# Loading q and k once each, four projection products of 192 columns, and a rewritten order for the first head: an attention and mixture-of-experts kernel on one core

## The chip, the cores and the metric

The kernel runs on one core of a Trainium2 chip. The metric is the device time of one execution in microseconds (us); lower is better. The engines are named as in the profile: PE (matrix products) with its weight loads PEld, DVE (vector), ACT (scalar, activations), POOL (GpSimd) and SP (the queue that issues most DMA transfers).

## The reference, cut to what matters

```python
# q, k, v: (2, 8, 768, 64); proj: (64, 6)
q_bits = (einsum('bhsd,dk->bhsk', q, proj) > 0)      # 6 sign bits for each row
k_bits = (einsum('bhsd,dk->bhsk', k, proj) > 0)
mask   = q_bucket[:, :, :, None] == k_bucket[:, :, None, :]    # bucket = the 6 bits as a number
scores = where(mask, scale * q @ k.T, -1e9)
attn   = softmax(scores);  x = attn @ v              # 16 heads
x = moe(x)       # each token: its best of 8 experts, relu(x @ w1) @ w2, times two gates
out = elu(x @ w_in) @ w_out
```

## The kernel before, in words

Attention runs head by head (16 heads of 768 rows and 64 dimensions), then comes the routing of the tokens, the expert layers and a last feed-forward block. The change is in the attention alone.

**One head.** q and k arrive transposed, 64 dimensions on the partitions, 768 rows along the free axis. Each is loaded twice, to partitions 0 to 63 and to 64 to 127 of `raw` (`load_qk`, L402; four DMAs a head). `project` (L1143) multiplies the 64 low partitions by `proj_w`: four products of 384 columns, each to its own 32 partitions of PSUM bank `bank_a` (q first half, q second half, k first half, k second half). `sign` (L841, DVE) turns this into 0/1 `bits`. `code` (L1159, PE) multiplies the bits by the +1/-1 `pat_bf`, once for q (c=0) and once for k (c=1), 384 columns each; a bucket matches where the sum equals a popcount. `mask_even` (L847, DVE) and `mask_odd` (L627, ACT) write this match as 64 more rows of the operands `q_a` and `k_a`, so that the score product itself gives about 2^60 less where buckets differ. The products are made of a high part (rounded to fp32r) and a low part (the rest): `high` (L823, DVE) rounds q and k into `q_b` and `k_b`; POOL scales k in `raw` (L532), copies the high parts to the top of `q_a` and `k_a` (L505, L514) and subtracts for the low parts (L507, L516). `scores` (L1168) is four products for one tile of 128 rows, tile m to `pair_s` or `pair_t`.

**The order of the work.** Every engine has its order written out by hand, in groups n; a head has three groups (part = 0, 1, 2), each with two score tiles. In group n PE makes `scores` of tiles m_s and m_s+1, and transposes the exponentials (`turn_exps`, L1184) of tiles m_e = m_s-2 and m_e+1, six 128x128 blocks each: three to the first bank of `pair_u`, which wait until ACT has copied the tile before (`copy_t0`, L647), and three to the second, which wait for DVE's copy (`copy_t1`, L855). Parts 0 and 1 also hold half of the product with v (`times_v`, L1195, 12 products), part 2 holds `last` (L1224) and `project` of the next head. Before the change `code(g, 0)` stands at the end of part 0 and `code(g, 1)` in part 1 between the first `turn_exps` and `times_v`.

DVE's order in a group is

```python
copy_t1(m_e - 1); row_max(m_s); row_max(m_s + 1); copy_t1(m_e)
# part 0: sign(g)      parts 0, 1: high(g + 1, part); mask_even(g, part)
# part 1: inverse(g - 2)
```

and ACT's is

```python
copy_t0(m_e - 1)       # part 0: copy_rows(g - 3)
copy_t0(m_e); exp_rows(m_s); exp_rows(m_s + 1)
# parts 0, 1: mask_odd(g, part)     part 1: copy_u(g - 2)
# heads 8 to 15, parts 0, 1: first_hi(g - 8, part)   (half a chunk of expert weights rounded)
```

**The first head.** Tiles 0 to 5 and their preparation are written out apart. PE bridges its waits with `warm_up` products (`WARM_UP = (7, 10)`, L1246): 7 before `project(0)`, 10 between `code(0, 1)` and `scores(0)`. SP issues q of head 0, proj, the pattern table `pat`, head 1, v, and the remaining constants `cst`; ACT issues k of head 0 (twice) and `first`.

Of the kernel before, what the change touches and what calls it, by code (L numbers as in the profile page):

```python
# [22 lines left out]
ALU = mybir.AluOpType  # L23
ACT = mybir.ActivationFunctionType
AX = mybir.AxisListType
F32 = mybir.dt.float32
# [29 lines left out]
HALF = S // 2  # L56
JH = J // 2
# [38 lines left out]
def constants():  # L96
# [12 lines left out]
    for x in range(2):  # L109
        for side in range(2):  # L110
            a = (2 * x + side) * BIT_K
            pattern[a:a + NBITS, x, side * BUCKETS:(side + 1) * BUCKETS] = 2.0 * bits - 1.0
# [17 lines left out]
def program(nc, q, k, v, proj, w_gate, w_ogate, w1, w2, w_in, w_out, const, out):  # L130
    with ExitStack() as ctx:
# [31 lines left out]
        with ExitStack() as att:  # L163
# [10 lines left out]
            raw = sb("raw", [P, 2, 2, S])  # L174
# [7 lines left out]
            pat_bf = sb("pat_bf", [P, 2, P], BF16)  # L182
            proj_w = sb("proj_w", [D, BIT_K])
# [100 lines left out]
        s_low = [[sem(f"s_low{i}{x}") for x in "qk"] for i in range(2)]  # L284
        s_vld = [sem(f"s_vld{i}") for i in range(4)]
        s_setup = sem("s_setup")
        s_hi, s_hid, s_hia = sem("s_hi"), sem("s_hid"), sem("s_hia")
        s_ks = sem("s_ks")
        s_lo = sem("s_lo")
        s_cp, s_cpk = sem("s_cp"), sem("s_cpk")  # L290
# [99 lines left out]
        def _(sp):  # L390
# [11 lines left out]
            def load_qk(g, n, to):  # L402
                sp.dma_start(raw[to, g % 2, n], (q, k)[n][g // H, g % H]).then_inc(
                    (s_raw if to == top else s_low)[g % 2][n], 16)

            def load_head(g):
                if g >= 2:
                    sp.wait_ge(s_bits, g - 1)
                if g == 2:
                    sp.wait_ge(s_lo, 2)  # L410
                if g >= 3:
                    sp.wait_ge(s_cp, prepared(g - 2))
                for n in range(2):
                    load_qk(g, n, top)
                    load_qk(g, n, low)
# [17 lines left out]
            sp.dma_start(cst[:, P:], const[:, P:]).then_inc(s_cst, 16)  # L433
# [11 lines left out]
            for g in range(2, HEADS):  # L445
                load_head(g)
                if g == 2:
                    load_gates()
# [25 lines left out]
        def _(pool):  # L474
# [26 lines left out]
            def place_q(g):  # L501

                pool.wait_ge(s_ks, g)
                pool.wait_ge(s_hia if g == 1 else s_hi, 2 if g == 1 else 2 * (g - 2) + 1)
                pool.tensor_copy(q_a[top, g % 3, :], q_b[top, g % 3, :].bitcast(F32)).then_inc(s_cp, 1)  # L505
                pool.wait_ge(s_cp, prepared(g - 1) + 1)
                pool.tensor_tensor(q_b[low, g % 3, :], raw[low, g % 2, 0, :], q_b[low, g % 3, :].bitcast(F32),  # L507
                                   ALU.subtract).then_inc(s_cp, 1)

            def place_k(g):  # L510

                pool.wait_ge(s_cp, prepared(g - 1) + 2)
                pool.wait_ge(s_hia if g == 1 else s_hi, 3 if g == 1 else 2 * (g - 2) + 2)
                pool.tensor_copy(k_a[top, g % 3, :], k_b[top, g % 3, :].bitcast(F32)).then_inc(s_cp, 1)  # L514
                pool.wait_ge(s_cp, prepared(g) - 1)
                pool.tensor_tensor(k_b[top, g % 3, :], raw[top, g % 2, 1, :], k_b[top, g % 3, :].bitcast(F32),  # L516
                                   ALU.subtract).then_inc(s_cp, 1)

            pool.wait_ge(s_pat, 16)
            pool.tensor_copy(pat_bf[:, :, :], pat[:, :, :]).then_inc(s_setup, 1)  # L520
            pool.wait_ge(s_setup, 1)
            pool.wait_ge(s_hia, 1)
            pool.tensor_copy(k_a[top, 0, :], k_b[top, 0, :].bitcast(F32)).then_inc(s_cpk, 1)
            pool.wait_ge(s_cpk, 1)
            pool.wait_ge(s_hid, 1)
            pool.tensor_copy(q_a[top, 0, :], q_b[top, 0, :].bitcast(F32)).then_inc(s_cp, 1)

            pool.wait_ge(s_cp, prepared(0))
            for g in range(1, HEADS):
                pool.wait_ge(s_raw[g % 2][1], 16 * (g // 2 + 1))  # L530
                pool.wait_ge(s_low[g % 2][1], 16 * (g // 2 + 1))
                pool.tensor_scalar(raw[:, g % 2, 1, :], raw[:, g % 2, 1, :], SCALE, None, ALU.mult).then_inc(s_ks, 1)  # L532
# [93 lines left out]
        def _(act):  # L626
            def mask_odd(g, c):  # L627
                act.wait_ge(s_code, 2 * g + c + 1)
                if c == 0:
                    act.activation(q_a[D:P, g % 3, HALF:S], code_bank(g, c)[D:P, 0:HALF], ACT.Identity,  # L630
                                   bias=minus_pop[D:P, :]).then_inc(s_mk, 1)
                else:
                    act.activation(k_a[D:P, g % 3, HALF:S], code_bank(g, c)[D:P, 0:HALF], ACT.Relu, scale=BIG,
                                   bias=unmatched[D:P, :]).then_inc(s_mk, 1)
# [81 lines left out]
            act.activation(q_b[:, 1, :], raw[:, 1, 0, :], ACT.Copy).then_inc(s_hia, 1)
            act.wait_ge(s_ks, 1)
# [782 lines left out]
```

## Time and profile before

| | us |
|---|---|
| median of 3 runs | 791.83 (790.86 to 794.01) |
| the profiled execution's own time | 792.07 |
| its span, first to last instruction | 790.3 |
| PE busy | 766.2 (97%) |
| DVE busy | 440.8 (56%) |
| POOL busy | 374.3 (47%) |
| ACT busy | 352.7 (45%) |

Attention takes about the first 262 us, routing some 16, the expert layers up to about 540 and the last block the rest. Busy time of PE is that of pipelined products whose ends are modelled, so it says that products are in flight, not that PE could do no more. In the rows below a timeline line reads: start in us from the span's start, duration in us, engine, source line, operation, written tile <- read tiles, shapes, count merged into the line, and in brackets the idle time in front of it and what ended it.

### The profile page before, as it was taken

Reading aid. Unit: us, or ns where it says so; the run is one execution under the profiler, and the core shown is the slowest. Engines: PE = TensorE matmul, PEld = TensorE weight load, DVE = VectorE, ACT = ScalarE, POOL = GpSimd, SP = SyncE. Lnnn points to the kernel's source line nnn. Section 1 sums busy time; section 2 is a strip of 40 time slices with the busy share of each in tenths; the row PEclk is TensorE's granted clock in tenths of the full one; section 3 lists DMA queues with packets and bytes.
Section 4 is the critical chain, followed back from the end, with each engine's and each line's share of the span. In section 5 each row is a group of like instructions: output and inputs, shape, how many; then the busy total and the mean of one; then the engine's idle time right before and its main releaser. Section 6 shows DMA issues by size and latency. Waiting matters only on the chain.

```text
span 790.3 us, 12377 instructions
## 1 busy us (share of the span) xinstructions
PE 766.2 (97%) x4237; PEld 628.2 (79%) x4237; DVE 440.8 (56%) x776; ACT 352.7 (45%) x658; POOL 374.3 (47%) x258
## 2 busy tenths in 40 slices
PE   6899999999999999999999999999999999999997
PEld 3667776676667678888888888899899889989985
DVE  4877877777766664454444544669337316613720
ACT  4666767777776242134422340057227206503610
POOL 5855565677752289797777982134210010000000
PEclk9999999999999999999999999999999999999999
DMA  7524334223110187577565650430010020000000
GB/s 198 155 83 127 99 115 135 62 71 81 41 41 12 42 315 252 189 240 223 172 203 177 240 160 27 166 128 0 28 54 1 4 64 13 2 14 27 1 13 27
DMA packets 42234, 79.08 MB, mean 100 GB/s; under 512 B 19200, under 2 KB 21504, under 8 KB 42176
## 3 DMA queue, kind: packets, MB, share of 16 engines
q1 hardware_dynamic: 29280, 35.09, 15.3%
q10 hardware_dynamic: 9456, 31.92, 12.3%
q0 software_dynamic: 3440, 11.28, 4.4%
q8 instruction: 38, 0.62, 0.3%
q14 instruction: 20, 0.16, 0.1%
HBM read 66.99 MB, written 11.28 MB: 99 GB/s over the span
## 4 chain that ended last, share of the span: by engine, by line
PE 59%; issue 28%; DVE 4%; POOL 4%; ACT 2%; DMA 1%; POOLq 0%; SPq 0%; DVEq 0%
PE pair_s L1369 13%; PE pair_t L1384 13%; PE pair_u L1191 8%; PE bank_b L1206 7%; PE pair_s L1180 4%; PE pair_t L1180 3%; PE pair_u L1348 2%; PE bank_b L1228 1%; PE bank_a L1155 1%; POOL out L605 1%; PE pair_s L1421 1%; DVE g_lo L1132 1%; POOL y_raw L599 1%; DMA pat<-in_const 1%; ACT w_part L696 1%
## 5 line engine op out<-in xcount | busy, mean ns | idle before, releaser
L477 POOL TENSOR_TENSOR w_part<-w_raw,w_part 128x1024 fp32r<-128x1024 f32 x80 | 190.2, 2405 | 56.8 <-ACT w_part L702 56.7
L702 ACT ACTIVATE w_part<-w_raw 128x1024 fp32r<-128x1024 f32 x72 | 73.8, 1055 | 133.6 <-PE pair_t L1384 101.0
L1471 PE MATMUL pair_t<-w_part,g_hi 128*128 128x512 f32 x384 | 119.0, 391 | 0.3 <-POOL w_part L477 0.3
L605 POOL DMA_INDIRECT out<-o_sb,token x12 | 11.8, 984 | 208.5 <-DVE o_sb L1102 208.5
L1369 PE MATMUL pair_s<-w_part,xs_t 128*128 x456 | 108.7, 394 | 0.4 <-DVE xs_t L1010 0.4
L1384 PE MATMUL pair_t<-w_part,hid_t 128*128 x456 | 109.0, 394 | 0.0
L1369 PEld LDWEIGHTS pair_s<-w_part,xs_t 128*128 128x128 f32 x456 | 84.3, 188 | 17.6 <-issue 0.8
L1384 PEld LDWEIGHTS pair_t<-w_part,hid_t 128*128 128x128 f32 x456 | 84.4, 189 | 16.8
L794 ACT ACTIVATE elu<-elu 128x384 f32<-128x384 f32 x64 | 33.6, 524 | 123.3 <-DVE elu L1122 123.1
L1191 PEld LDWEIGHTS pair_u<-first,exps 128*128 128x128 f32 x564 | 62.7, 140 | 32.4 <-ACT exps L643 18.6
L1191 PE MATMUL pair_u<-first,exps 128*128 128x128 f32 x564 | 81.0, 278 | 6.0 <-ACT exps_t L652 4.6
L1471 PEld LDWEIGHTS pair_t<-w_part,g_hi 128*128 128x128 f32 x384 | 71.6, 188 | 15.1 <-issue 0.7
L1471 PE MATMUL pair_t<-w_part,g_lo 128*128 128x512 f32 x192 | 74.9, 390 | 0.0
L1421 PE MATMUL pair_u<-y_t,w_part 128*128 128x384 f32 x384 | 69.3, 334 | 0.3 <-DVE elu L1127 0.3
L1421 PE MATMUL pair_s<-y_t,w_part 128*128 128x384 f32 x384 | 69.3, 335 | 0.0
L652 ACT ACTIVATE exps_t<-pair_u 128x384 f32<-128x384 f32 x94 | 46.0, 489 | 49.9 <-PE pair_u L1191 49.6
L1421 PEld LDWEIGHTS pair_u<-y_t,w_part 128*128 128x128 f32 x384 | 66.8, 188 | 0.7 <-DVE elu L1127 0.6
L1421 PEld LDWEIGHTS pair_s<-y_t,w_part 128*128 128x128 f32 x384 | 66.9, 188 | 0.2
L860 DVE COPY exps_t<-pair_u 128x384 f32<-128x384 f32 x94 | 51.8, 552 | 23.8 <-PE pair_u L1191 23.4
L1028 DVE CAST hid_t<-pair_u 128x512 fp32r<-128x512 f32 x38 | 26.1, 686 | 67.2 <-PE pair_u L1348 67.2
L1206 PE MATMUL bank_b<-exps_t,v_nat 128*64 128x384 f32 x336 | 60.4, 494 | 0.0
L838 DVE TENSOR_REDUCE nmax<-pair_s 128x1 f32<-128x768 f32 x48 | 45.8, 954 | 18.9 <-PE pair_s L1180 17.5
(204 smaller groups left out, 1171.3 us busy)
## 6 DMA issues: line engine op xcount, KB each, us to landing
w_raw<-in_moe_w ACTq DMA_DIRECT2D x48, 512.0 KB, 6.4
w_raw<-in_moe_w SPq DMA_DIRECT2D x16, 512.0 KB, 5.3
raw<-in_q SPq DMA_DIRECT2D x32, 192.0 KB, 3.4
raw<-in_k SPq DMA_DIRECT2D x30, 192.0 KB, 3.7
ys_sorted<-ys SPq DMA_DIRECT2D x19, 256.5 KB, 3.9
w_raw<-in_moe_w_in ACTq DMA_DIRECT2D x8, 512.0 KB, 5.6
v_nat<-in_v SPq DMA_DIRECT2D x16, 192.0 KB, 2.4
x_rows<-rows_sb SPq DMA_DIRECT2D x32, 96.0 KB, 2.9
```

The lines of the kernel that those rows point to most:

```text
L477: pool.tensor_tensor(chunk_of(w_part, n, 1, c), w_raw[n % 2][c][:, :], chunk_of(w_part, n, 0, c).bitcast(F32), ALU.subtract).then_inc(s_wl ...
L652: act.activation(turned_tile(m, slice(0, JH)), exps_pair(m)[:, 0, 0:HALF].rearrange("p (j n) -> p j n", j=JH), ACT.Copy).then_inc(s_t0, 1)
L702: act.activation(chunk_of(w_part, n, 0, c), w_raw[n % 2][c][:, :], ACT.Copy).then_inc(s_whi, 1)
L838: dve.tensor_reduce(nmax[:, g % 2, qt:qt + 1], score_pair[m % 2][:, :, 0:HALF], AX.XY, ALU.max, negate=True).then_inc(s_mx, 1)
L860: dve.tensor_copy(turned_tile(m, slice(JH, J)), exps_pair(m)[:, 1, 0:HALF].rearrange("p (j n) -> p j n", j=JH)).then_inc(s_t1, 1)
L1180: mm = pe.matmul(score_pair[m % 2][:, h, 0:HALF], a[:, g % 3, t], b[:, g % 3, h * HALF:(h + 1) * HALF], start=first, stop=not first)
L1191: mm = pe.transpose(exps_pair(m)[:, part, n * P:(n + 1) * P], exps[:, m % 4, kt * P:(kt + 1) * P], ident)
L1206: mm = pe.matmul(u_bank(u)[o * D:(o + 1) * D, 0:HALF], v_nat[:, (u - 1 + o) % 4, j, :], turned_half(2 * u - 1 + o)[:, j], start=j == 0, st ...
L1369: mm = pe.matmul(pair_s[:, h, :], xs_t[:, xp, c * P:(c + 1) * P], w_part[:, bass.ds(par, 1), wp, a:a + 512], start=c == 0 and xp == 0 and ...
L1384: mm = pe.matmul(pair_t[:, s % 2, :], hid_t[:, hp, c * P:(c + 1) * P], w_part[:, bass.ds(par, 1), wp, a:a + DM], start=c == 0 and n == 0, ...
L1421: mm = pe.matmul(hidden_bank[n % 4][:, 0:NB], w_in_p[:, wp, c, f * P:(f + 1) * P], y_t[:, yp, c, :], start=c == 0 and m == 0, stop=c == CD ...
L1471: mm = pe.matmul(pair_t[:, t % 2, :], gp[:, f, j * P:(j + 1) * P], w_out_p[:, wp, f, :], start=f == 0 and m == 0, stop=f == FT - 1 and m == 2)
```

## The change

- **Loads.** q goes only to partitions 0 to 63 of `raw`, k only to 64 to 127: two DMAs a head instead of four. `cst` is issued after head 2's loads instead of before them. ACT issues proj, twice, and SP both loads of head 0.
- **Projection.** `proj_w` now has 128 partitions (q's weights in columns 0 to 5, k's in 6 to 11), and `project` makes four products of 192 columns with q and k at once. `sign` handles 192 columns. `code` becomes two products of 192 columns with two patterns; the masks write two runs of 192 with a gap.
- **Order.** `code(g, 1)` moves to the end of part 1 on PE. `mask_odd(g, 0)` and `mask_even(g, 0)` move from the end of part 0 into part 1, behind the first copy. `first_hi` moves ahead of `copy_t0(m_e)`. POOL reads k from the high partitions and writes across halves.
- **First head.** ACT prepares k_a, the patterns and q_a, and scales k for heads 1 and 2 (`scale_k`), which POOL did; a tiny activation stands in front. DVE rounds both operands of heads 0 and 1. `WARM_UP` and all of the work after attention stay as they are.

```diff
-            def load_qk(g, n, to):
-                sp.dma_start(raw[to, g % 2, n], (q, k)[n][g // H, g % H]).then_inc(
-                    (s_raw if to == top else s_low)[g % 2][n], 16)
+            def load_qk(g, n):
+                sp.dma_start(raw[(top, low)[n], g % 2], (q, k)[n][g // H, g % H]).then_inc(s_raw[g % 2][n], 16)
...
                 if g == 2:
-                    sp.wait_ge(s_lo, 2)
+                    sp.wait_ge(s_lo, 1)
+                    sp.wait_ge(s_qa, 1)
+                    sp.wait_ge(s_ka, 1)
+                    sp.wait_ge(s_cp, prepared(0))
...
-            load_qk(0, 0, top)
-            sp.wait_ge(s_zero, 2)
-            sp.dma_start(proj_w[:, 0:NBITS], proj).then_inc(s_proj, 16)
-            load_qk(0, 0, low)
+            load_qk(0, 0)
+            load_qk(0, 1)
             sp.dma_start(pat[:, :, :], const[:, slice(*COL["pattern"])].rearrange("p (x n) -> p x n", x=2)).then_inc(s_pat, 16)
             load_head(1)
             load_v(0)
-            sp.dma_start(cst[:, P:], const[:, P:]).then_inc(s_cst, 16)
...
-                pool.tensor_tensor(q_b[low, g % 3, :], raw[low, g % 2, 0, :], q_b[low, g % 3, :].bitcast(F32),
+                pool.tensor_tensor(q_b[low, g % 3, :], raw[top, g % 2, :], q_b[top, g % 3, :].bitcast(F32),
...
-                pool.tensor_copy(k_a[top, g % 3, :], k_b[top, g % 3, :].bitcast(F32)).then_inc(s_cp, 1)
+                pool.tensor_copy(k_a[top, g % 3, :], k_b[low, g % 3, :].bitcast(F32)).then_inc(s_cp, 1)
...
-                pool.tensor_scalar(raw[:, g % 2, 1, :], raw[:, g % 2, 1, :], SCALE, None, ALU.mult).then_inc(s_ks, 1)
+                if g >= 3:
+                    pool.wait_ge(s_raw[g % 2][1], 16 * (g // 2 + 1))
+                    pool.tensor_scalar(raw[low, g % 2, :], raw[low, g % 2, :], SCALE, None, ALU.mult).then_inc(s_ks, 1)
...
+            act.dma_start(proj_w[0:D, 0:NBITS], proj).then_inc(s_proj, 16)
+            act.dma_start(proj_w[D:P, NBITS:2 * NBITS], proj).then_inc(s_proj, 16)
             act.dma_start(first[:, :], const[:, 0:P + 3]).then_inc(s_id, 16)
+            act.wait_ge(s_zero, 2)
+            act.activation(nmax[:, 0, 0:1], bits[:, QUART:QUART + 1], ACT.Copy)
             act.wait_ge(s_raw[0][1], 16)
+            act.activation(k_a[0:D, 0, :], raw[D:P, 0, :], ACT.Copy, scale=SCALE).then_inc(s_ka, 1)
+            act.wait_ge(s_pat, 16)
+            for h, at in enumerate((slice(0, D), slice(D, P))):
+                act.activation(pat_bf[at, h, :, :], pat[at, :, :], ACT.Copy).then_inc(s_setup, 1)
+            act.wait_ge(s_raw[0][0], 16)
+            act.activation(q_a[0:D, 0, :], raw[0:D, 0, :], ACT.Copy).then_inc(s_qa, 1)
             act.wait_ge(s_id, 16)
             mask_odd(0, 0)
             mask_odd(0, 1)
+            scale_k(1)
             exp_rows(0)
             exp_rows(1)
+            scale_k(2)
...
+                if g < HEADS and part == 1:
+                    mask_odd(g, 0)
+                if 8 <= g < 8 + NCH and part < 2:
+                    first_hi(g - 8, part)
                 if 0 <= m_e < J * HEADS:
                     copy_t0(m_e)
...
-                if g < HEADS and part < 2:
-                    mask_odd(g, part)
+                if g < HEADS and part == 1:
+                    mask_odd(g, 1)
...
-                dve.tensor_scalar(bits[:, :], bank_a[:, 0:HALF], 0.0, None, ALU.is_gt).then_inc(s_sgn, 1)
+                dve.tensor_scalar(bits[:, 0:QUART], bank_a[:, 0:QUART], 0.0, None, ALU.is_gt).then_inc(s_sgn, 1)
...
+            high(0, 0)
+            high(0, 1)
+            dve.wait_ge(s_hi, 2)
+            dve.scalar_tensor_tensor(k_b[0:D, 0, :], raw[D:P, 0, :], SCALE, k_b[D:P, 0, :].bitcast(F32),
+                                     ALU.mult, ALU.subtract).then_inc(s_lo, 1)
             sign(0)
+            mask_even(0, 0)
             mask_even(0, 1)
+            high(1, 0)
+            high(1, 1)
             row_max(0)
...
                     copy_t1(m_e - 1)
+                if g < HEADS and part == 1:
+                    mask_even(g, 0)
                 if m_s < J * HEADS:
                     row_max(m_s)
...
-                if g < HEADS and part < 2:
-                    mask_even(g, part)
+                if g < HEADS and part == 1:
+                    mask_even(g, 1)
...
-                    mm = pe.matmul(bank_a[i * BIT_K:(i + 1) * BIT_K, 0:HALF], proj_w[:, :],
-                                   raw[0:D, g % 2, i // 2, i % 2 * HALF:(i % 2 + 1) * HALF], start=True, stop=True)
+                    mm = pe.matmul(bank_a[i * BIT_K:(i + 1) * BIT_K, 0:QUART], proj_w[:, :],
+                                   raw[:, g % 2, i * QUART:(i + 1) * QUART], start=True, stop=True)
...
-                pe.matmul(code_bank(g, c)[:, 0:HALF], pat_bf[:, c, :], bits[:, :], start=True, stop=True).then_inc(s_code, 1)
+                for h in range(2):
+                    mm = pe.matmul(code_bank(g, c)[:, h * QUART:(h + 1) * QUART], pat_bf[:, h, c, :], bits[:, 0:QUART],
+                                   start=True, stop=True)
+                mm.then_inc(s_code, 1)
...
-                if g < HEADS and part == 1:
-                    code(g, 1)
...
                     turn_exps(m_e + 1)
-                if g < HEADS and part == 0:
-                    code(g, 0)
+                if g < HEADS and part < 2:
+                    code(g, part)
```

## Rows read from the trace of the kernel before

**Rows 1.** Chain that ended last: first score products of heads 3, 4, 8, 15 (start, duration).

```profile
41.58 0.89 PE pair_s L1180 x4
...
57.49 0.91 PE pair_s L1180 x4
...
117.09 0.90 PE pair_s L1180 x4
...
225.83 0.89 PE pair_s L1180 x4
```

**Rows 2.** Stretches of a middle and a late head: busy time of each engine, PE clock, DMA.

```profile
57.40:72.30 14.90, 14.90 (x104) 10.70 (x100) 11.55 (x19) 10.34 (x23) 8.70 (x9) 1.00 0.38 109
163.60:179.20 15.60, 15.07 (x105) 10.67 (x101) 11.55 (x19) 11.44 (x25) 11.30 (x10) 1.00 0.31 77
```

**Rows 3.** Timeline of the start, up to the first scores.

```profile
0.72 0.58 SPq L403 DMA_DIRECT2D raw<-in_q  x1
...
6.81 1.28 ACT L709 ACT_TABLE_LOAD   x1 [6.81 <-DMA raw<-in_k]
...
8.10 0.84 ACT L709 ACTIVATE k_b<-raw 128x768 fp32r<-128x768 f32 x1
...
9.26 0.10 PEld L1166 LDWEIGHTS bank_a<-bits,pat_bf 128*128 128x128 bf16 x1 [3.76 <-issue]
...
12.76 0.66 PEld L1180 LDWEIGHTS pair_s<-k_a,q_a 128*128 128x128 f32 x2 [0.17 <-issue]
```

**Rows 4.** DMA issues in the first 0.9 us: size, us from issue to landing.

```profile
raw<-in_q SPq DMA_DIRECT2D x1, 192.0 KB, 3.3
```

**Rows 5.** Timeline of tiles 4 to 6, where the second head is prepared.

```profile
22.32 0.56 DVE L831 CAST k_b<-raw 128x768 fp32r<-128x768 f32 x1 [2.30 <-POOL raw L532]
...
22.79 0.55 DVE L845 TENSOR_SCALAR bits<-bank_a 128x384 bf16<-128x384 f32 x1
...
23.39 0.10 PEld L1166 LDWEIGHTS bank_a<-bits,pat_bf 128*128 128x128 bf16 x1 [2.41 <-DVE bits L845]
...
27.70 0.30 PEld L1180 LDWEIGHTS pair_s<-k_a,q_a 128*128 128x128 f32 x2
```

**Rows 6.** Timeline of head 7: end of part 0, part 1, part 2.

```profile
102.12 0.30 PEld L1180 LDWEIGHTS pair_s<-k_a,q_a 128*128 128x128 f32 x2 [0.62 <-issue]
...
107.07 0.10 PEld L1166 LDWEIGHTS bank_a<-bits,pat_bf 128*128 128x128 bf16 x1
...
107.54 0.61 DVE L852 TENSOR_SCALAR q_a<-bank_a,first 64x384 fp32r<-64x384 f32 x1 [1.20 <-PE bank_a L1166]
...
111.44 0.61 DVE L852 TENSOR_SCALAR k_a<-bank_a,first 64x384 fp32r<-64x384 f32 x1
...
112.08 0.31 DVE L866 TENSOR_SCALAR den<-den 128x6 f32<-128x6 f32 x1
...
112.41 0.30 PEld L1180 LDWEIGHTS pair_s<-k_a,q_a 128*128 128x128 f32 x2
...
112.42 0.19 DVE L867 RECIPROCAL den<-den 128x6 f32<-128x6 f32 x1
...
113.42 0.96 DVE L838 TENSOR_REDUCE nmax<-pair_s 128x1 f32<-128x768 f32 x1
...
114.30 0.95 DVE L838 TENSOR_REDUCE nmax<-pair_t 128x1 f32<-128x768 f32 x1
```

**Rows 7.** The same head, end of part 2 and the next head's first scores.

```profile
115.16 0.55 DVE L860 COPY exps_t<-pair_u 128x384 f32<-128x384 f32 x1
...
115.28 0.79 PEld L1191 LDWEIGHTS pair_u<-first,exps 128*128 128x128 f32 x6
...
116.24 0.15 PEld L1155 LDWEIGHTS bank_a<-raw,proj_w 64*32 64x32 f32 x8 [0.17 <-issue]
...
117.02 0.30 PEld L1180 LDWEIGHTS pair_s<-k_a,q_a 128*128 128x128 f32 x2 [0.62 <-issue]
```

**Rows 8.** A late head, part 1: PE in front of the first transposes.

```profile
170.89 0.64 PEld L1191 LDWEIGHTS pair_u<-first,exps 128*128 128x128 f32 x6 [0.81 <-issue]
```

**Rows 9.** POOL's groups of instructions over four middle heads: busy us, mean ns, idle before.

```profile
L516 POOL TENSOR_TENSOR k_b<-raw,k_b 64x768 fp32r<-64x768 f32 x4 | 7.4, 1839 | 0.3
...
L505 POOL CAST q_a<-q_b 64x768 fp32r<-64x768 f32 x4 | 3.3, 818 | 13.5 <-DVE q_b L831 13.5
```

More of the change, by code:

```diff
@@ L56 @@
 HALF = S // 2
+QUART = S // 4
 JH = J // 2
@@ L109, in constants @@
     for x in range(2):
-        for side in range(2):
-            a = (2 * x + side) * BIT_K
-            pattern[a:a + NBITS, x, side * BUCKETS:(side + 1) * BUCKETS] = 2.0 * bits - 1.0
+        for quart in range(4):
+            a, to = quart * BIT_K + x * NBITS, quart % 2 * BUCKETS
+            pattern[a:a + NBITS, x, to:to + BUCKETS] = 2.0 * bits - 1.0
     put("pattern", pattern.reshape(P, 2 * P))
@@ L409, in load_head @@
                 if g == 2:
-                    sp.wait_ge(s_lo, 2)
+                    sp.wait_ge(s_lo, 1)
+                    sp.wait_ge(s_qa, 1)
+                    sp.wait_ge(s_ka, 1)
+                    sp.wait_ge(s_cp, prepared(0))
                 if g >= 3:
                     sp.wait_ge(s_cp, prepared(g - 2))
-                for n in range(2):
-                    load_qk(g, n, top)
-                    load_qk(g, n, low)
+                load_qk(g, 0)
+                load_qk(g, 1)
                 if g >= 6:
@@ L447, in _ @@
                 if g == 2:
+                    sp.dma_start(cst[:, P:], const[:, P:]).then_inc(s_cst, 16)
                     load_gates()
@@ L746, in _ @@
                     copy_t0(m_e + 1)
-                if g < HEADS and part < 2:
-                    mask_odd(g, part)
+                if g < HEADS and part == 1:
+                    mask_odd(g, 1)
                 if g >= 2 and part == 1:
                     copy_u(g - 2)
-                if 8 <= g < 8 + NCH and part < 2:
-                    first_hi(g - 8, part)
             copy_u(HEADS)
@@ L830, in high @@
                     dve.wait_ge(s_sc, J * (g - 2))
-                dve.tensor_copy((q_b, k_b)[c][:, g % 3, :], raw[:, g % 2, c, :]).then_inc(s_hi if g else s_hid, 1)
+                to = (q_b, k_b)[c][at, g % 3, :]
+                if c == 1 and g == 0:
+                    dve.tensor_scalar(to, raw[at, 0, :], SCALE, None, ALU.mult).then_inc(s_hi, 1)
+                else:
+                    dve.tensor_copy(to, raw[at, g % 2, :]).then_inc(s_hi, 1)
             def row_max(m):
@@ L1161, in code @@
                 if g == 0:
[L1162 removed]
+                    pe.wait_ge(s_setup, 2)
                 if g >= 2 and c == 1:
@@ L1173, in scores @@
                 if g == 0:
-                    pe.wait_ge(s_lo, 2)
+                    pe.wait_ge(s_lo, 1)
+                    pe.wait_ge(s_qa, 1)
+                    pe.wait_ge(s_ka, 1)
                 if m >= 2:
```

82 lines of the change are left out of this document (34 added, 48 removed).

## The prediction

> **What bounds the kernel now.** I read the chain that ended last first. Inside attention it runs through PE almost alone. It gives the head periods: heads 4 to 7 take (117.09 - 57.49) / 4 = 14.90 us each, heads 8 to 14 (225.83 - 117.09) / 7 = 15.53 us, head 3 takes 57.49 - 41.58 = 15.91 us [rows 1]. The table of stretches then says why: in a middle head PE has products in flight for 14.90 of 14.90 us, while DVE is busy 11.55, ACT 10.34 and POOL 8.70; in a late head PE has gaps (15.07 of 15.60) [rows 2]. So in the middle PE's own work and order set the pace, and anything that makes PE wait is paid in full. The timeline shows three places where PE waits: until the first scores at 12.76 [rows 3], 2.41 us at tile 4, for `sign(1)` on DVE, which stands behind `high(2,1)`, which waited for POOL's scaling of k [rows 5], and 0.81 us in part 1 of each late head, where a middle head shows 0.17: `mask_odd` and `first_hi` stand in front of `copy_t0` on ACT [rows 8]. Nothing after attention is touched, so I carry its shift one to one to the end.
>
> **The first head.** Old: `code(0,0)` starts at 9.26 and scores at 12.76, 3.50 later, the time of the codes and the ten warm-up products [rows 3]. New: q is issued at 0.72 and landed 3.3 later before [rows 3, 4]; k is now SP's second issue, 0.6 later, so it lands at about 4.6 (estimate). Behind it on DVE: `high(0,1)` 0.56 as its like in [rows 5], the subtraction of 768 elements about 0.96 (as a maximum over 768 takes, [rows 6]), `sign(0)` with half of the columns about 0.35 of the 0.55 in [rows 5]. With starts between them that is 6.6, and code starts at 6.7. `project(0)` lies beside the subtraction: 0.78 at full clock [rows 7], at the start at most twice that, so it ends before 6.3. The pattern copies on ACT (256 elements each, about half of the 0.84 for 768 in [rows 3]) end at about 6.4, just under the cover; if they ran over, code would be late by as much. The warm-up products still lie between: scores(0) at 6.7 + 3.5 = 10.2, so 2.5 us earlier. The masks end near 8.6 and q's low part on POOL (1.84, [rows 9]) near 6.5, both covered by the warm-up. If k lands at 4.0 or at 6.0, the gain is 3.1 or 1.1.
>
> The table load of ACT, 1.28 us and on the spot followed by the activation at 8.10 [rows 3], now comes in front of the landing and leaves the path; I count nothing for it, since it stood beside DVE and POOL work. The Trainium skill ("ScalarE: Activation LUTs", What ACT_TABLE_LOAD costs) gives 1.28 us plus a drain of 1.38; the trace agrees with the first and shows no such drain behind it. By the skill's figure ACT would be ready some 0.5 us after k lands, which moves the pattern copies to the edge of the path.
>
> **Tiles 0 to 5.** `scale_k(2)` on ACT now stands behind exp_rows(1) and ends before DVE comes to `high(2,1)`, so the 2.41 us go [rows 5]. I give 0.3 back: ACT's 0.84 in front of exp_rows(2), four code products for two, and tile 5 then waits for exp_rows(3). Tile 6 was at 27.70 [rows 5], and should be at 27.70 - 2.5 - 2.4 + 0.3 = 23.1: **-4.6 us**. `cst` lands later, but its first reader on POOL stands before head 2's operands, due only at tile 12.
>
> **Steady head, PE's work.** `project` to the next scores takes 117.02 - 116.24 = 0.78 [rows 7]. The columns halve; it can save between nothing (issue-bound) and 0.39. I take 0.32, since the gap in [rows 7] reads as products draining. Two codes of 192 columns cost what one of 384 did, within 0.05. From the first scores to the code in a part without a code between it is 107.07 - 102.12 = 4.95 [rows 6]; part 1 now has that form, so `code(g,1)` comes at C = 107.07 + 0.15 + 4.95 = 112.17, where the scores of part 2 stood at 112.41: -0.24.
>
> **Steady head, the new wait.** `mask_even(g,1)` used to run at 111.44; now it can't before the code at C is through, and it stands in front of DVE's whole part 2: `inverse`, `copy_t1(m_e-1)`, two maxima and `copy_t1(m_e)`, for which PE's second three transposes wait. Starts from C: mask +0.47 (107.07 to 107.54), den +0.64 (111.44 to 112.08), reciprocal +0.34, copy +0.10 (estimate from its 0.19), maximum +0.47 (the copy's 0.55 less the 0.08 by which maxima overlap), second maximum +0.88, copy +0.87, its 0.55 and 0.05 to PE [rows 6, 7]: C + 4.37. From the second three transposes to `project` it is 0.96 - 0.40 = 0.56 [rows 7]. So from C to project is 4.93, where before from 112.41 to 116.24 it was 3.83 [rows 6, 7]: **+1.10**. Before, the copy ended at 115.71 and PE came to it at about 115.68 [rows 7]: no slack was left to take this up. ACT's `mask_odd` has the same wait, but its chain (mask, copy_u, copy_t0) lets PE go at C + 2.06 and is passed by DVE's. Moving `mask_even(g,0)` into part 1 costs nothing: it only changes places with `copy_t1`.
>
> New period: 14.90 - 0.24 + 1.10 - 0.32 = 15.44, +0.54 a head. In late heads `copy_t0` now comes before mask and `first_hi`, so their extra 0.63 (15.53 - 14.90) goes, and `first_hi` lies in ACT's idle time: 15.53 to 15.44, -0.09. Head 3 has three casts of constants that delayed it by 15.91 - 14.90 = 1.01 [rows 1]; with `mask_even(g,0)` gone from part 0 they run in DVE's wait: +0.54 - 1.01 = -0.47. Head 2: +0.54 less 0.10 for the shorter sign: +0.44. Head 15 has no project: +1.10 - 0.24 - 0.63 = +0.23.
>
> **Sum.** -4.6 (start), +0.44 (head 2), -0.47 (head 3), 4 x 0.54 = +2.16 (heads 4 to 7), 7 x -0.09 = -0.63, +0.23: -2.9 us. The profiled execution had 792.07, near the median 791.83, so 789.2. Within 0.5% (788 to 796) is about what this kernel's measurement can't tell from no change.
>
> Two DMAs a head fewer count nothing: the DMA engines are busy 0.38 of a middle head [rows 2]. POOL's waits on its own counts (s_x, s_wlo) are for its own earlier instructions, and it idled 13.5 us in four heads in front of L505 alone [rows 9].
>
> **Rivals.**
> (a) The new wait doesn't bind, because DVE has more room than these starts give. For it: DVE is busy only 11.55 of 14.90 [rows 2]. Against: the copy at 115.16 was already due [rows 7]. It takes 14 x 1.10 = 15.4 off: 773.8. Half hidden it is 781.
> (b) Slower: POOL's three instructions that now cross from one half of the partitions to the other take much longer. A late head has 11.30 of POOL work [rows 2], of which these are 2 x 1.84 + 0.82 = 4.5 [rows 9]. POOL sets the pace when it passes 15.44, that is from 1.92 times their duration; at 2.5 times it is 18.05 a late head, +2.6 x 7, and 8.70 + 6.75 = 15.45 in a middle one: 789.2 + 18.3 = 807. It ends beyond 796 from 2.13 times on. No row shows such an instruction on POOL. The Trainium skill ("GPSIMD Engine Reference", Architecture) says that for ordinary compute each of the eight cores owns its own 16 partitions, which speaks for this rival; no row here bears on it, as all of POOL's instructions before stay in their half.
> (c) The start gains only the 2.4 of the scaling, as k lands late behind the other transfers or the patterns run over: -0.4 in sum, 791.7.
>
> **Chances.** My forecast 0.55, (a) wholly or in half 0.17, (b) 0.12, (c) 0.16. My own case carries the unknowns: project 0 to 0.39 saved (13 heads, up to +4.2 or -0.9), the wait 0.8 to 1.3 (-4.2 to +2.8), the start 3.2 to 5.2: 784 to 795, of which 0.20 below 788, 0.33 within, 0.02 above. (a) is all faster; (b) 0.10 slower, 0.02 same; (c) 0.13 same, 0.03 slower. Faster 0.37, same 0.48, slower 0.15. Range 781 to 795.5: it takes in (c) and the half of (a).
>
> **What would show it.** The first scores at about 10.2, no wait of 2 us in front of the second head's code, tile 6 near 23; first scores of heads 3 to 8 some 15.4 apart and of late heads too; DVE idle for over 1 us in front of `mask_even(g,1)` at the end of part 1, and PE's second three transposes in part 2 released by DVE's copy; project to scores about 0.46. I am wrong if heads are under 15 us (rival a) or POOL's L507, L514, L516 are well over 1.84 and 0.82 us (rival b).

## The result: the changed kernel is slower

| | before | after |
|---|---|---|
| median, us | 792.92 (790.86 to 794.03, 4 runs) | 800.57 (800.36 to 800.65, 4 runs) |
| span of the profiled execution, us | 790.3 | 798.7 |

The ratio is 1.0099, 95% interval 1.0074 to 1.0124: slower by 7.7 us, where 2.9 us less were forecast. 800.57 lies above the range of 781 to 795.5.

**Where the time went.** The chain of the changed kernel that ended last, the first score products of heads 3, 4, 8 and 15 (start, duration):

```profile
39.99 0.91 PE pair_s L1202 x4
56.13 0.89 PE pair_s L1202 x4
...
120.86 0.89 PE pair_s L1202 x4
...
234.20 0.91 PE pair_s L1202 x4
```

Heads are numbered as in [rows 1], by the g of the groups: in head g's groups head g is prepared and the tiles of head g-1 are scored. Head 2 is the stretch from tile 6 to the first row here.

| stretch | before | after | change | forecast |
|---|---|---|---|---|
| up to tile 6 | 27.70 | 25.13 | -2.57 | -4.6 |
| head 2 | 13.88 | 14.86 | +0.98 | +0.44 |
| head 3 | 15.91 | 16.14 | +0.23 | -0.47 |
| heads 4 to 7 | 4 x 14.90 | 4 x 16.18 | +5.13 | +2.16 |
| heads 8 to 14 | 7 x 15.53 | 7 x 16.19 | +4.60 | -0.63 |
| all up to head 15 | | | +8.37 | -3.1 |

The start gained about half of what it should, and each steady head lost 0.75 us more than it should. What follows the first scores of head 15 is 0.0 (forecast +0.23). Of the 11.3 us between forecast and result (8.4 more by the two profiled executions, for 2.9 less), 9.4 lie in heads 2 to 14 and 2.0 in the start.

**The steady head.** The chain of waits of the changed kernel, from the code of part 1 of one head to the next head's scores:

```profile
114.96 0.18 PE bank_a L1184 x2
...
115.16 0.61 DVE k_a L865
...
115.80 1.14 DVE den L879
...
117.08 0.53 DVE exps_t L873
117.61 0.67 DVE nmax L850
...
118.39 0.95 DVE nmax L850
119.33 0.47 DVE exps_t L873
...
119.85 0.55 PE pair_u L1213 x3
120.40 0.46 PE bank_a L1172 x8
120.86 0.89 PE pair_s L1202 x4
```

It is the chain of the prediction, step by step: code, `mask_even`, the two instructions of `inverse`, copy, two maxima, copy, PE's second three transposes, `project`, scores. In [rows 6, 7] the same stretch ran on PE. One step has another size. The add on `den` (L879), six elements to a partition, takes 1.14 us, where it took 0.31 in [rows 6]. (Here and below a duration in the chain can differ by some hundredths from the timeline's.) The timeline of the changed kernel says what stands beside it:

```profile
114.69 0.21 PEld L1184 LDWEIGHTS bank_a<-bits,pat_bf 128*128 128x128 bf16 x2
...
115.07 1.84 POOL L515 TENSOR_TENSOR k_b<-raw,k_b 64x768 fp32r<-64x768 f32 x1
...
115.16 0.61 DVE L865 TENSOR_SCALAR k_a<-bank_a,first 64x384 fp32r<-64x384 f32 x1 [1.13 <-PE bank_a L1184]
...
115.80 1.13 DVE L879 TENSOR_SCALAR den<-den 128x6 f32<-128x6 f32 x1
```

POOL's subtraction runs from 115.07 to 116.91, and the add, begun at 115.80, ends at 116.93, 0.02 after it. In [rows 6] the add stood at 112.08, and POOL's subtraction began at 112.44, behind it. Counted from the head's first scores, POOL's subtraction has hardly moved (10.32 us behind them before, 10.48 now), while the add has gone from 9.96 to 11.21. From the code at C = 114.69 to the second transposes it is 5.16, forecast 4.37. `mask_even` at 115.16, which reads PSUM, keeps its 0.61 beside the same subtraction.

**The start.** The timeline of the changed kernel up to the first scores, and at tiles 2 to 6:

```profile
4.67 1.81 POOL L519 TENSOR_TENSOR q_b<-raw,q_b 64x768 fp32r<-64x768 f32 x1 [4.23 <-DVE q_b L843]
...
4.82 2.08 DVE L841 TENSOR_SCALAR k_b<-raw 64x768 fp32r<-64x768 f32 x1 [0.24 <-DMA raw<-in_k]
...
8.21 0.13 PEld L1184 LDWEIGHTS bank_a<-bits,pat_bf 128*128 128x128 bf16 x2 [2.63 <-DVE bits L857]
...
11.71 0.66 PEld L1202 LDWEIGHTS pair_s<-k_a,q_a 128*128 128x128 f32 x2 [0.17 <-issue]
...
14.72 1.82 POOL L515 TENSOR_TENSOR k_b<-raw,k_b 64x768 fp32r<-64x768 f32 x1
...
15.30 1.66 DVE L843 CAST q_b<-raw 64x768 fp32r<-64x768 f32 x1
...
20.90 0.11 PEld L1184 LDWEIGHTS bank_a<-bits,pat_bf 128*128 128x128 bf16 x2 [1.29 <-DVE bits L857]
...
25.13 0.30 PEld L1202 LDWEIGHTS pair_s<-k_a,q_a 128*128 128x128 f32 x2
```

k has landed at 4.8 (forecast 4.6). But `high(0,1)` takes 2.08 us where 0.56 was counted: POOL had begun the low part of q 0.15 us before it, and `high(0,1)` ends 0.42 after POOL. So the code comes at 8.21 and not at 6.7, and the first scores at 11.71 and not at 10.2 ([rows 3]: 12.76). The two casts for the third head (g = 2) meet POOL in the same way, q's at 15.30 (1.66) and k's at 19.19 (1.27 beside a subtraction begun at 18.20). `sign(1)` stands behind them, so 1.29 us of the wait of 2.41 at tile 4 [rows 5] stay.

### The profile page after: what moved, and what is told of

The parts are those of the page before. It is cut to its first block, busy times and chain, and to the rows that moved or that the text cites. A ratio compares the mean times of both kernels' runs of the same rounds, so it can differ in the third digit from the quotient of the medians.

```text
span 798.7 us, 12417 instructions
## 1 busy us (share of the span) xinstructions
PE 766.0 (96%) x4269; PEld 630.2 (79%) x4269; DVE 452.0 (57%) x783; ACT 353.8 (44%) x661; POOL 368.8 (46%) x254
## 4 chain that ended last, share of the span: by engine, by line
PE 54%; issue 28%; DVE 12%; POOL 2%; ACT 1%; DMA 1%; POOLq 0%; SPq 0%; DVEq 0%
PE pair_s L1389 13%; PE pair_t L1404 13%; PE bank_b L1228 7%; PE pair_u L1213 6%; DVE nmax L850 4%; PE pair_s L1202 3%; PE pair_t L1202 3%; PE pair_u L1368 2%; DVE exps_t L873 2%; DVE den L879 2%; DVE k_a L865 1%; POOL out L601 1%; PE pair_s L1441 1%; DVE g_lo L1148 1%; PE bank_a L1172 1%
## 5 line engine op out<-in xcount | busy, mean ns | idle before, releaser
L1213 PE MATMUL pair_u<-first,exps 128*128 128x128 f32 x564 | 85.6, 279 | 15.9 <-DVE exps_t L873 12.0
L1404 PEld LDWEIGHTS pair_t<-w_part,hid_t 128*128 128x128 f32 x456 | 84.4, 188 | 16.9
```

The source lines that it names most:

```text
L1213: mm = pe.transpose(exps_pair(m)[:, part, n * P:(n + 1) * P], exps[:, m % 4, kt * P:(kt + 1) * P], ident)
L1404: mm = pe.matmul(pair_t[:, s % 2, :], hid_t[:, hp, c * P:(c + 1) * P], w_part[:, bass.ds(par, 1), wp, a:a + DM], start=c == 0 and n == 0, ...
```

## The experiments

Theory A: a cast or add of DVE that works in SBUF, or a DVE instruction with two inputs there, and an instruction of POOL exclude each other; the one that began first goes on, the other lasts longer. With the late `code(g,1)`, which puts DVE's part 2 on PE's path, this makes the loss. In every run of a changed kernel the edit is against the changed kernel, if nothing else is said; a ratio is to the kernel before, run in the same series.

**1. inverse ahead of the masks (part 1).**

```diff
                 if g + 1 < HEADS and part < 2:
                     high(g + 1, part)
+                if part == 1 and g >= 2:
+                    inverse(g - 2)
                 if g < HEADS and part == 1:
                     mask_even(g, 1)
...
-                if part == 1 and g >= 2:
-                    inverse(g - 2)
```

> The changed kernel, with inverse(g-2) put ahead of mask_even(g,1), into the time in which DVE waits for code(g,1). Theory A (den's first instruction, 1.14 us instead of 0.31, is held back by POOL's subtraction L515 beside it, and stands in DVE's chain to copy_t1): the instruction falls to about 0.3, it leaves the chain with the reciprocal, 1.15 + 0.10 less in each head; head period 16.19 to 14.9, in sum 14 x 1.26 = 17.6 less: 783. Rival B (the order on PE and ACT costs the time, not DVE's chain): the period stays within 0.3 of 16.19, 797 to 801. Rival C (the instruction is long by itself, wherever it stands): it still takes 1.1, but leaves the chain: 783 too, told from A by its duration.

Measured: 784.25 us (782.45 to 784.48); to the kernel before (792.09) 0.9891, interval 0.987 to 0.9911. In its chain the first scores of heads 4, 8 and 15 stand at 53.48, 113.26 and 217.86: 14.94 a head, 1.24 less than 16.18: the add and the reciprocal held DVE for 117.08 - 115.80 = 1.28 in the chain above. At its new place (122.67) the add takes 0.17, so it isn't long by itself (rival C). The reciprocal keeps its 0.19 although it begins 0.10 after POOL's cast of 0.82: it isn't held. Two instructions of six elements cost 16 us in all.

**2. code(g,1) at its old place on PE, nothing else.**

```diff
                     turn_exps(m_e + 1)
+                if g < HEADS and part == 1:
+                    code(g, 1)
                 if g == 2 and part == 1:
...
-                if g < HEADS and part < 2:
-                    code(g, part)
+                if g < HEADS and part == 0:
+                    code(g, 0)
```

> The changed kernel with code(g,1) put back where it was before the change, between the first transposes of part 1 and times_v; all else as changed. Theory A (the late code holds mask_even(g,1), and with it DVE's part 2): the whole wait goes, 1.9 us a head, and what is left is PE's work less the 0.32 of the projection: period 14.5 in middle and late heads, 14 x 1.7 = 23 less: 777. Rival B (the moved masks of q, or POOL's operations across halves, cost it): the period stays over 15.5, 790 or more.

Measured: 778.64 (778.2 to 779.23), ratio 0.9826 (0.9809 to 0.9843). Heads 4 to 7 and 8 to 14 take 14.53 each. 22 us faster than the changed kernel: the whole loss of the steady heads hangs on this move. Its timeline at the end of part 1:

```profile
106.02 0.82 POOL L513 CAST k_a<-k_b 64x768 fp32r<-64x768 f32 x1 [2.68 <-DVE k_b L843]
...
106.56 0.31 DVE L879 TENSOR_SCALAR den<-den 128x6 f32<-128x6 f32 x1
...
106.92 1.84 POOL L515 TENSOR_TENSOR k_b<-raw,k_b 64x768 fp32r<-64x768 f32 x1
...
107.70 0.96 DVE L850 TENSOR_REDUCE nmax<-pair_s 128x1 f32<-128x768 f32 x1
```

Even this add of 0.31 is held: POOL's cast ends at 106.84, the add at 106.87, and without POOL beside it it takes 0.17 (experiments 1 and 3). The maximum behind it reads PSUM and keeps 0.96 beside the subtraction.

**3. POOL's subtraction of k waits until inverse is done** (from head 3 on); DVE's own order is left.

```diff
                 pool.wait_ge(s_cp, prepared(g) - 1)
+                if g >= 3:
+                    pool.wait_ge(s_inv, g - 2)
                 pool.tensor_tensor(k_b[top, g % 3, :], raw[low, g % 2, :], k_b[low, g % 3, :].bitcast(F32),
```

> The changed kernel with DVE's order untouched, but POOL's subtraction L515 waits until DVE's reciprocal of the same part is through, so it no longer runs beside den's first instruction. Theory A (the pair collides): that instruction falls from 1.14 to 0.31, as before the change, and the period by 0.83, to 15.36, near the 15.44 of the prediction; 14 x 0.83 = 11.6 less: 789. Rival C (the instruction is long because of what stands in front of it on DVE): it keeps 1.14, the period stays 16.19, 800 or somewhat over.

Measured: 787.47 (786.66 to 788.31), ratio 0.9934 (0.9915 to 0.9952). The chain's part 2 is as it was, with one step changed (timeline of this kernel):

```profile
111.43 0.17 DVE L881 TENSOR_SCALAR den<-den 128x6 f32<-128x6 f32 x1
...
111.98 1.82 POOL L517 TENSOR_TENSOR k_b<-raw,k_b 64x768 fp32r<-64x768 f32 x1 [1.35 <-DVE den L882]
```

The add takes 0.17 instead of 1.13, and the period is 15.22 instead of 16.18, in both 0.96 less. This is the test that tells the hold from the length of the chain: the same work in the same order on DVE, and POOL alone made to wait. That the time comes near the 789.2 of the prediction is in part luck: by head 3 this kernel had gained 2.2 us where 4.2 were forecast, and heads 3 to 14 gained 1.6 where a loss of 1.1 was forecast.

The same timeline shows a limit of theory A. POOL's scaling of k doesn't keep DVE out for its whole length:

```profile
148.40 2.22 POOL L530 TENSOR_SCALAR raw<-raw 64x768 f32<-64x768 f32 x1
...
149.39 0.54 DVE L845 CAST q_b<-raw 64x768 fp32r<-64x768 f32 x1
```

The cast began 0.99 us behind POOL, took no longer than alone and ended 0.69 before it; POOL's 2.13 became 2.22. It is so in heads 10 to 14 of this run. Why the middle of the scaling is open was not tested.

**4. POOL's first subtraction behind DVE's own.**

```diff
             pool.wait_ge(s_hi, 1)
+            pool.wait_ge(s_lo, 1)
             pool.tensor_tensor(q_b[low, 0, :], raw[top, 0, :], q_b[top, 0, :].bitcast(F32), ALU.subtract).then_inc(s_cp, 1)
```

> The changed kernel, with POOL's first subtraction (q of head 0, at 4.67 in the changed kernel) held until DVE's k_b subtraction is done. Theory A: DVE's scaling of k, 2.08 us beside it, falls to about 0.56, code(0,0) comes at 6.7 instead of 8.21, the first scores at 10.2 instead of 11.71, 1.5 less in sum: 799.1. Rival D (the scaling is slow by itself, as a product on 64 partitions, or waits for the landing): it keeps 2.0, no change: 800.6.

Measured: 797.35 (797.1 to 798.7), ratio 1.0066 (1.0047 to 1.0085): 3.2 less than the changed kernel, twice the 1.5 expected. The timeline:

```profile
4.76 0.56 DVE L842 TENSOR_SCALAR k_b<-raw 64x768 fp32r<-64x768 f32 x1 [0.47 <-DMA raw<-in_k]
...
6.46 1.81 POOL L520 TENSOR_TENSOR q_b<-raw,q_b 64x768 fp32r<-64x768 f32 x1 [6.02 <-DVE k_b L886]
...
10.12 0.54 PEld L1203 LDWEIGHTS pair_s<-k_a,q_a 128*128 128x128 f32 x2 [0.17 <-issue]
...
13.22 0.55 DVE L844 CAST q_b<-raw 64x768 fp32r<-64x768 f32 x1
13.28 2.19 POOL L515 TENSOR_TENSOR k_b<-raw,k_b 64x768 fp32r<-64x768 f32 x1
...
22.04 0.30 PEld L1203 LDWEIGHTS pair_s<-k_a,q_a 128*128 128x128 f32 x2
```

The first scores at 10.12, forecast 10.2. The second half of the gain is in the last rows: here DVE's cast began 0.06 before POOL's subtraction, kept 0.55, and POOL's row is longer; in the changed kernel POOL was first, and the cast took 1.66. The second cast, at 16.82, then comes before POOL's next instruction and takes 0.56 instead of 1.27. Tile 6 comes at 22.04, forecast 23.1.

**5. The same, but POOL waits for `high(0,1)` only** (`pool.wait_ge(s_hi, 2)` in place of 1), so that it meets DVE's two-input subtraction.

> GpSimd's first subtraction waits for VectorE's high(0,1) but not for its subtraction low(0,1), so it starts during that subtraction, which has two inputs in SBUF. In the run in which it waits for both, 797.35 us, high(0,1) took 0.56 and the first scores began at 10.12. Theory A (an instruction of VectorE in its quick form, or with two inputs in SBUF, and one of GpSimd exclude each other, and the one that began first goes on): VectorE's subtraction begins first and keeps its 0.95; GpSimd's shows about 1.81 + 0.7 = 2.5 us in its row, and ends where it did, near 8.2; the time is the same, 797.4. Rival (two-input instructions do not exclude GpSimd's, only the quick forms do): GpSimd's row keeps 1.81 and ends near 7.4; the time is again the same. The time tells nothing here, the row tells.

Measured: 798.41 (797.19 to 800.52), ratio 1.0081 (1.0061 to 1.0101), span 795.4 beside 795.6 in experiment 4. The timeline:

```profile
5.52 0.95 DVE L885 SCALAR_TENSOR_TENSOR k_b<-raw,k_b 64x768 fp32r<-64x768 f32 x1
5.57 2.58 POOL L519 TENSOR_TENSOR q_b<-raw,q_b 64x768 fp32r<-64x768 f32 x1 [5.13 <-DVE k_b L841]
```

DVE was first by 0.05 and kept its 0.95; POOL's 1.81 became 2.58, and it ended 8.15 - 6.47 = 1.68 after DVE did. So instructions with two inputs in SBUF take part, and the one held may be POOL's. The time was to be that of experiment 4, and the equal spans don't show it: at tile 2 POOL was first (13.45 before 13.85), tile 6 came at 23.14, and the first scores of head 15 at 232.17 against 231.13. The work behind them, which is the same in both kernels, was 1.2 us shorter in this execution.

**6. inverse at the end of part 2** (`part == 2` for `part == 1` in front of `inverse(g - 2)`, at its place).

> VectorE's inverse(g-2), the add and the reciprocal, is issued at the end of part 2 of the group and no longer at the end of part 1; nothing else is moved. Theory A: the chain behind code(g,1) loses the add with its hold (1.13) and the reciprocal (0.19); the period falls from 16.18 to 14.9 to 15.0, as it did with the inverse ahead of mask_even(g,1) (14.94), and the time is 784 (782 to 786). If GpSimd's scaling multiply, which has one input in SBUF and runs then, holds VectorE too, the add shows more than 0.31 there as well; if only its subtractions do, it shows 0.1 to 0.3. Rival (the order of the chain does not matter, the kernel has become slower for the loads): 800.

Measured: 784.19 (784.05 to 784.38), ratio 0.9894 (0.9878 to 0.991), 14.93 a head. The gain is that of experiment 1. In most heads the add misses POOL's scaling (at 112.37 it began 0.20 before it and kept 0.16), but the first time it doesn't:

```profile
36.09 2.13 POOL L528 TENSOR_SCALAR raw<-raw 64x768 f32<-64x768 f32 x1
...
37.70 0.54 DVE L879 TENSOR_SCALAR den<-den 128x3 f32<-128x3 f32 x1
```

The add (0.17 alone in experiment 1) ends at 38.24, 0.02 behind the scaling. So POOL's instruction with one input holds DVE too, here in its last part; experiment 3 shows its middle free. The next add, begun at 52.63, 0.37 behind the next scaling, takes 0.48 and ends 1.28 before that scaling does.

**7. The order alone, on the kernel before**: masks, `first_hi` and `code(g,1)` at their new places; loads, `high`, projection and first head old.

> The kernel before with the order moves alone: code(g,1) behind the second three transposes of part 1, the masks' first halves and first_hi at their new places. Both halves are still loaded twice, high has the 96-partition form as before, the projection is as before and so is the first head. Theory A: the projection and the loads gain little, so this shows nearly all the loss by itself. From the steady sum: the project term (-0.32) and the part 1 term (-0.24) fall away, the held add (+0.83) comes with the order: heads 4 to 7 take 14.90 + 1.10 + 0.83, about 16.5 to 16.9, heads 8 to 14 about 16.2 to 16.9; from 12 late and early heads of 1 to 1.9 us more, 807 (800 to 813). Rival (the new loads and casts make the loss, the order is harmless): 786 to 793.

Measured: 806.09 (805.65 to 807.2), ratio 1.0172 (1.0154 to 1.019), 16.38 a head. That is a little under the 16.5 to 16.9 expected: `code(g,1)` comes 10.04 us behind the head's first scores here too (108.92 to 118.96), so the -0.24 of part 1 belongs to the order and should have stayed in the sum. The order loses 13.6 us; the new loads, projection and first head then win 5.5 of it back (806.09 - 800.57): 43.52 - 39.99 = 3.5 by head 3, and 0.2 in each of the heads after it.

**8. Three mends together**: 1, 2 and 4 on the changed kernel.

> The changed kernel with three mends: code(g,1) again ahead of the groups that wait for VectorE's copies, inverse(g-2) ahead of mask_even(g,1), GpSimd's first subtraction behind VectorE's first. Theory A: code(g,1) early alone gave 778.64 with a period of 14.53, in which VectorE's chain no longer ends a wait; so the inverse adds nothing to it, and the later first subtraction takes off the 3.2 us that it took off by itself: 775.4 (774 to 777). Rival (the mends add up: -16.3, -21.9 and -3.2 from 800.57): 759.

Measured: 776.89 (776.72 to 777.28), ratio to before 0.9801 (0.9788 to 0.9815), 14.54 a head. It has the lowest median of all runs, 3% under the changed kernel. A table of stretches shows PE's products in flight again through the whole head (engines as in [rows 2]):

```profile
95.08:109.61 14.53, 14.53 (x104) 10.86 (x103) 11.38 (x20) 10.33 (x24) 8.95 (x9) 1.00 0.33 92
```

The changed kernel's head shows 1.1 us in which PE has none, and DVE busier by 0.74:

```profile
104.66:120.84 16.18, 15.09 (x104) 10.79 (x103) 12.12 (x20) 10.33 (x23) 8.97 (x8) 1.00 0.29 83
```

Against experiment 2 it gains 1.75 and not 3.2: at tile 2 POOL was first again (timeline of this kernel), and tile 6 came at 23.59, not 22.04.

```profile
13.36 1.82 POOL L515 TENSOR_TENSOR k_b<-raw,k_b 64x768 fp32r<-64x768 f32 x1
14.07 1.54 DVE L844 CAST q_b<-raw 64x768 fp32r<-64x768 f32 x1
```

**9. The three mends, with `first_hi` last in the group again.**

```diff
-                if 8 <= g < 8 + NCH and part < 2:
-                    first_hi(g - 8, part)
...
                     copy_u(g - 2)
+                if 8 <= g < 8 + NCH and part < 2:
+                    first_hi(g - 8, part)
```

> The kernel of the three mends (776.89 us, period 14.54 in all heads) with one part of ScalarE's new order undone: first_hi is again the last work of ScalarE in a group. In the kernel before, heads 8 to 14, which have a first_hi, took 15.53 each and heads 4 to 7 14.90. Theory A: that 0.63 a head comes back in heads 8 to 14 and nothing else changes: 776.9 + 7 x 0.63 = 781.3 (780 to 782.5), with heads 4 to 7 still at 14.54. Rival (the late heads in before were long for another reason, the masks or the loads): 777, with all heads at 14.54.

Measured: 777.38 (777.23 to 778.09), ratio 0.9805 (0.9788 to 0.9822); 14.53 in heads 4 to 7, 14.62 in heads 8 to 14. My expectation fell: moving `first_hi` alone is worth 0.08 a late head, not 0.63.

**10. ScalarE's and VectorE's order alone, on the kernel before**: experiment 7 with `code(g,1)` at its early place.

> The kernel before with ScalarE's new order alone: code(g,1) stays at its early place, the loads, the 96-partition high, the projection and the first head are as before; first_hi and the masks' first halves are at their new places. Theory A: heads 4 to 7 keep 14.90 and heads 8 to 14 fall from 15.53 to it, so 792.5 - 7 x 0.63 = 788.1 (786.5 to 789.5); what is left to the 776.9 of the three mends, 11 us, is then the new start (12.76 to 10.2, and the wait behind tile 4) and 0.36 a head for the projection. Rival (the gain of the mended kernel is all in the order): 777 to 780.

Measured: 785.02 (784.74 to 785.13), ratio 0.9899 (0.9882 to 0.9915). Heads 4 to 14 take 14.81 each: 0.72 off each late head, 0.09 off each of heads 4 to 7, and head 3 takes 14.81 for 15.91, since the three casts of constants no longer stand behind a mask. That last 1.1, which the prediction had (1.01), I had left out of this expectation.

**11 and 12. The three mends, with `mask_odd(g,0)` back at the end of part 0 (11), and with `first_hi` back too (12).** The edit of 11; 12 adds that of 9.

```diff
-                if g < HEADS and part == 1:
-                    mask_odd(g, 0)
...
-                if g < HEADS and part == 1:
-                    mask_odd(g, 1)
+                if g < HEADS and part < 2:
+                    mask_odd(g, part)
```

> The kernel of the three mends (776.89 us, 14.54 a head throughout) with ScalarE's mask_odd(g,0) again behind the exponentials of part 0, in every head, and first_hi left at its new place. Moving first_hi back alone cost only 0.08 a late head. Theory B, formed from that: a late head of the kernel before was longer because mask_odd(g,0), which waits for the code, and first_hi (0.63) stood one behind the other ahead of the next group's copy_t0, so either move alone takes the 0.63 away; then this one shows 14.5 to 14.65 in all heads and 777.0 to 777.8. Theory C: the mask's place does it alone, so the mask back brings 0.6 a late head: 781.3.

> The same with both put back, mask_odd(g,0) and first_hi, so that ScalarE's order in the groups is wholly that of the kernel before. Theories B and C both expect the late heads' 0.63 back, and nothing in heads 4 to 7: late heads at 15.1 to 15.2, 776.9 + 7 x 0.63 = 781.3 (780 to 782.5). Rival D: the 0.63 of the kernel before came from something else that the new loads have taken away (the second halves, the wider casts on VectorE), and the order of ScalarE's work brings nothing: 777 to 778.

Measured: 777.66 (777.02 to 778.45), ratio 0.9811 (0.9786 to 0.9836), for 11, and 782.2 (781.3 to 783.45), ratio 0.9862 (0.9836 to 0.9888), for 12. Late heads take 14.58 in 11 and (216.95 - 110.38) / 7 = 15.22 in 12, whose heads 4 to 7 keep 14.59. Theory B holds (the mask and `first_hi` one behind the other in front of the next copy make the 0.63): either move alone takes it away, both back bring it back. The timeline of 12 shows the pile in front of the copy, which runs from 132.20:

```profile
130.95 0.58 ACT L629 ACTIVATE q_a<-bank_a,first 64x384 fp32r<-64x384 f32 x1 [1.07 <-PE bank_a L1183]
131.56 0.63 ACT L697 ACTIVATE w_part<-w_raw 128x512 fp32r<-128x512 f32 x1
...
132.81 0.64 PEld L1212 LDWEIGHTS pair_u<-first,exps 128*128 128x128 f32 x6 [0.79 <-issue]
```

## Why the prediction was wrong

**The step that failed** is the chain of the new wait, at "den +0.64 (111.44 to 112.08), reciprocal +0.34". The 0.34 was the add's duration (and the gap behind it) at another moment, when POOL had not yet begun its subtraction, and it was itself held: in the kernel before POOL's cast runs from 111.54 to 112.36, the add ends at 112.39, and alone it takes 0.17. By moving `code(g,1)` I moved `mask_even` and so the add 1.25 us later in the head, into that subtraction. The step measured 1.17 (115.80 to 116.97). That is +0.83 on each head, and with 14.90 - 0.24 + 1.10 + 0.83 - 0.32 the sum gives 16.27, measured 16.18. Experiment 3 takes just this away and finds 15.22 a head and 787.47 in all. In head 15 POOL has no next head to prepare, and the add takes 0.17 (at 245.34).

**The same mistake at the start**: "`high(0,1)` 0.56 as its like in [rows 5]", while the same paragraph let POOL's subtraction end "near 6.5", that is, run beside it, and called it covered. Covered on its own engine it was; it held DVE for 1.5 us. Experiment 4 gives the first scores at 10.12 and tile 6 at 22.04.

The trace of before had the sign, in rows that I did not use. Its timeline at the casts of constants:

```profile
46.76 1.84 POOL L507 TENSOR_TENSOR q_b<-raw,q_b 64x768 fp32r<-64x768 f32 x1
...
47.56 1.12 DVE L913 CAST tri_bf<-cst 128x128 bf16<-128x128 f32 x1
48.60 0.21 DVE L914 CAST ones_bf<-cst 128x128 bf16<-128x128 f32 x1
48.74 0.21 DVE L915 CAST iota_bf<-cst 128x128 bf16<-128x128 f32 x1
```

Three casts of the same size, 1.12, 0.21 and 0.21 us; the long one ends with POOL's subtraction (48.68 and 48.60). It isn't long for being the first: in experiment 10 the first two take 0.22 and the third, begun 0.05 behind POOL's cast, takes 0.85. And at the scaling:

```profile
29.68 2.13 POOL L532 TENSOR_SCALAR raw<-raw 128x768 f32<-128x768 f32 x1
31.38 0.84 DVE L831 CAST q_b<-raw 128x768 fp32r<-128x768 f32 x1
```

0.84 instead of 0.56 beside a one-input instruction of POOL. The Trainium skill states the rule ("SBUF — State Buffer", SBUF: two separate sides): VectorE and GpSimd share a port pair; a VectorE instruction in a two-port mode, or one with two inputs in SBUF (this one only against a GpSimd instruction that reads SBUF), and a GpSimd instruction exclude each other for the whole instruction, and whichever starts first has it. Experiments 3, 4 and 5 agree, with 1.13 against 0.17, 2.08 against 0.56, and 2.58 against 1.81 us. For POOL's scaling "the whole instruction" isn't what was measured: in experiment 3 a cast of 0.54 ran in its middle.

**What was right.** That PE's order sets the pace, that the late code turns DVE's part 2 into its wait, and at which transposes: the chain above, and experiment 2 (-22 us from one move). `project` to scores 0.46 (120.40 to 120.86 in the chain), forecast 0.46. k's landing, 4.8 for 4.6. The -0.24 of part 1: the late code comes 10.10 behind the head's first scores (104.59 to 114.69), forecast 10.05. Late heads no longer differ from middle ones (16.19 and 16.18). Head 3's gain from the constants: about 1.1 in experiment 10.

**Right in size, half right in cause.** The 0.63 of the late heads I put down to `first_hi` and the mask together; it needs both, and either move takes it (experiments 9, 11, 12).

**The rivals.** (a), the wait doesn't bind: it does, 14.53 without it, 16.18 with it. (b), POOL's instructions across the halves take longer: they don't, by the groups of the changed kernel over four middle heads, which answer to [rows 9]:

```profile
L515 POOL TENSOR_TENSOR k_b<-raw,k_b 64x768 fp32r<-64x768 f32 x4 | 7.3, 1835 | 0.3
...
L513 POOL CAST k_a<-k_b 64x768 fp32r<-64x768 f32 x4 | 3.3, 821 | 10.7 <-DVE k_b L843 10.7
```

Slower came by a way that was none of my rivals. (c), a start that gains only 2.4, is near what happened (2.57), for another reason than late transfers.

**What stays open.** Why the first scores start a little faster in some runs than in others (in experiment 4 two products took 0.79, in experiment 8 and in the changed kernel 1.09), though the granted clock reads 1.00 in all three. By the rows this decides who is first at tile 2: DVE's cast comes 0.85 later in experiment 8 than in 4, POOL's subtraction only 0.08. Whether DVE and POOL can be kept apart there for good wasn't tried. Open too: why POOL's scaling lets a cast of DVE through in its middle, and why the work behind attention took 1.2 us less in the profiled execution of experiment 5 than in that of experiment 4.

## What to carry to other kernels

A duration read in a trace belongs to its moment: before it is moved, ask what POOL does at the old time and at the new one, and look for twins of one instruction with different durations. Short adds and casts of DVE on SBUF are the ones to place with care, since a hold costs them what is left of POOL's instruction, whatever their own size. In these runs DVE instructions that read PSUM, and reciprocals, were not held. A product that others wait for should not be moved behind work on its own engine only because its result is needed late: what stands behind the consumer on the other engine becomes due with it.

## What the runs showed of the hardware that was not expected

- The hold doesn't scale with the held instruction: six elements to a partition, 0.17 us alone (experiment 3), stand 1.13 us beside a subtraction of 1.84.
- 0.06 us decide who is held: 13.22 before 13.28 gave DVE's cast 0.55 us (experiment 4), begun 0.71 after POOL's it took 1.54 (experiment 8).
- POOL's subtraction and cast that read partitions 64 to 127 and write 0 to 63 take 1835 and 821 ns, as within a half (1839 and 818, [rows 9]). Its scaling takes 2.13 us on 64 partitions in the changed kernel as on 128 before.
- Which instructions are held: DVE's casts, its add and its two-input subtraction. Its reciprocal in SBUF kept 0.19 us inside a cast of POOL (experiment 1, 122.88 to 123.07 in 122.78 to 123.60).
- POOL's scaling (2.13 us) holds DVE in its last part (experiment 6, 0.54 for 0.17) and not in its middle (experiment 3, 0.54 for 0.54).
